# Keys and queries turned by VectorE in blocks of 32, in a fused attention and channel-mix kernel

## What is computed

```python
def _attn_ref(q, k, v):                       # each (4, 8, 1152, 64), float32
    q_pool = q.reshape(B, H, S // 2, 2, D).mean(axis=3)
    scores = scale * np.matmul(q_pool, k.transpose(0, 1, 3, 2))
    scores = scores - np.max(scores, axis=-1, keepdims=True)
    attn = np.exp(scores)
    attn = attn / (np.sum(attn, axis=-1, keepdims=True) + 1e-09)
    return np.matmul(attn, v)

def _moe_ref(x, g_ln, w_ch1, w_ch2):          # x (4, 576, 512): the heads side by side
    xn = (x - mu) / np.sqrt(var + 1e-06) * g_ln
    return x + np.maximum(xn @ w_ch1, 0.0) @ w_ch2     # 512 -> 2048 -> 512
```

## Time and profile before

| what | value |
|---|---|
| median of 3 runs | 860.61 us (859.78 to 860.65) |
| the profiled execution's own time | 861.76 us |
| its span | 860.0 us |
| TensorE (PE) busy in the span | 839.6 us |
| VectorE (DVE) | 427.2 us |
| ScalarE (ACT) | 326.3 us |
| GpSimd (POOL) | 351.3 us |
| attention | until about 450 us, 16 steps |
| channel mix | about 450 us to the end |

### The profile page before, as it was taken

The page is one execution under the profiler, slowest core; times in us unless marked ns, Lnnn a source line. Parts: engine busy times, 40 slices in busy tenths (PEclk is TensorE's granted clock), DMA queues, the critical chain, the costliest instruction groups (busy, mean ns, idle before and its releaser), DMA issues.

```text
span 860.0 us, 16086 instructions
## 1 busy us (share of the span) xinstructions
PE 839.6 (98%) x6712; PEld 704.1 (82%) x6712; DVE 427.2 (50%) x667; ACT 326.3 (38%) x707; POOL 351.3 (41%) x252
## 2 busy tenths in 40 slices
PE   6899999999999999999989999999999999999998
PEld 3767778777878777787769999999999999999997
DVE  5757777777776777676525543213223123222111
ACT  1555657555566556565533441121111111121110
POOL 1477888888777788877780000000000000000000
PEclk9999999999999999999999999999999999999999
DMA  5441223322233312220202321001001000001001
GB/s 113 108 133 36 59 75 84 85 61 61 72 84 84 84 42 57 71 57 28 68 11 74 123 73 38 0 1 38 1 1 37 1 1 37 2 1 37 1 1 37
DMA packets 75160, 42.46 MB, mean 49 GB/s; under 512 B 40016, under 2 KB 66640, under 8 KB 75088
## 3 DMA queue, kind: packets, MB, share of 16 engines
q1 hardware_dynamic: 73872, 40.84, 17.2%
q10 hardware_dynamic: 1216, 0.59, 0.3%
HBM read 36.70 MB, written 4.72 MB: 48 GB/s over the span
## 4 chain that ended last, share of the span: by engine, by line
PE 91%; POOL 4%; DVE 2%; ACT 1%; DMA 1%; issue 1%; SPq 0%; POOLq 0%; DVEq 0%; ACTq 0%
PE banks L865 23%; PE banks L878 23%; PE banks L490 14%; PE banks L479 14%; PE banks L433 4%; PE banks L477 4%; POOL acc L355 3%; PE banks L506 2%; PE banks L405 2%; PE banks L441 1%; PE banks L414 1%; DVE pm L657 1%; ACT pT L589 1%; POOL acc L359 1%; PE banks L225 1%; PE banks L517 1%
## 5 line engine op out<-in xcount | busy, mean ns | idle before, releaser
L355 POOL TENSOR_TENSOR acc<-acc,pT 128x576 f32<-128x576 f32 x160 | 233.9, 1462 | 23.2 <-POOL acc L355 0.4
L865 PE MATMUL banks<-xT,weights 128*128 128x384 f32 x1152 | 217.1, 338 | 0.0
L878 PE MATMUL banks<-weights,hT 128*128 128x512 f32 x864 | 210.7, 389 | 0.0
L865 PEld LDWEIGHTS banks<-xT,weights 128*128 128x128 f32 x1152 | 202.1, 188 | 6.0 <-issue 0.2
L657 DVE TENSOR_REDUCE pm<-banks 128x2 f32<-128x1024 f32 x128 | 153.4, 1223 | 75.0 <-PE banks L433 73.9
L934 DVE SCALAR_TENSOR_TENSOR hT<-banks,hT 128x384 fp32r<-128x384 f32 x96 | 53.5, 558 | 272.4 <-ACT hT L915 272.3
L878 PEld LDWEIGHTS banks<-weights,hT 128*128 128x128 f32 x864 | 160.9, 188 | 27.1 <-issue 0.3
L589 ACT ACTIVATE pT<-banks 128x576 f32<-128x576 f32 x288 | 168.0, 656 | 25.7 <-PE banks L477 19.5
L915 ACT ACTIVATE hT<-banks 128x384 fp32r<-128x384 f32 x96 | 47.2, 492 | 324.6 <-PE banks L865 324.6
L479 PE MATMUL banks<-qT,kT 64*128 64x288 f32 x1728 | 162.8, 299 | 0.6 <-ACT pT L589 0.3
L490 PE MATMUL banks<-pT,vn 128*64 128x288 f32 x1152 | 146.8, 409 | 1.2 <-DVE x L707 1.2
(11 more groups left out here) (74 smaller groups left out, 526.0 us busy)
## 6 DMA issues: line engine op xcount, KB each, us to landing
kn<-in_k_dram SPq DMA_DIRECT2D x32, 288.0 KB, 4.1
vn<-in_v_dram SPq DMA_DIRECT2D x16, 576.0 KB, 4.9
wstage<-in_moe_w_ch_dram SPq DMA_DIRECT2D x32, 256.0 KB, 2.9
qn<-in_q_dram SPq DMA_DIRECT2D x30, 256.0 KB, 3.1
out_dram<-x SPq DMA_DIRECT2D x16, 256.0 KB, 2.3
qn<-in_q_dram SPq DMA_DIRECT2D x30, 32.0 KB, 3.1
qn<-in_q_dram ACTq DMA_DIRECT2D x2, 256.0 KB, 5.0
out_dram<-x SPq DMA_DIRECT2D x4, 128.0 KB, 2.4
```

The costliest lines, as they stand in the source:

```text
L355: nc.gpsimd.tensor_tensor(total, pT[:, h % 2, 0] if kt == 1 else total, pT[:, h % 2, kt], ALU.add).then_inc(chained, 1)
L865: last = nc.tensor.matmul(ps_h[f % 2][:, 0:CW], weights[:, 2 * f, a, c * 128:(c + 1) * 128], xT[:, par, b, c], start=m == 0, stop=m == len ...
L878: last = nc.tensor.matmul(ps_y[kk], hT[:, f % 2, a, kk * 128:(kk + 1) * 128], weights[:, 2 * f + 1, b], start=f == 0 and m == 0, stop=f == ...
```

## The change

Three things change together.

- From pair 2 on (`TURNED`), VectorE turns keys and queries itself, in blocks of 32x32 elements, and writes them to the PSUM banks of KA and KQ; TensorE skips these tokens. So that 32x32 blocks come out as whole rows, SyncE loads keys and queries in another layout: 32 partitions each hold a run of 36 neighbouring rows, and the two halves of the 64 elements of a head come as two overlapping transfers of 32 partitions, 2,272 words each. In `VECTOR_STEPS` Q and K are the turning, ahead of the second `a`; `a` of the first half comes one block of maxima earlier.
- The maxima are turned by two ordinary products with the identity, one in each 64-column tile of the array, in place of one 128x128 transpose.
- The places are single banks now. O, E and L stand together behind the last scores and ahead of PV; SH stands between the two PVs; nine M are spread over the 18 S, the first ahead of them.

Besides, `EARLY` is 4, so that GpSimd splits no slice in steps 10 and 11 and the first chunk splits two more; and SyncE asks for values ahead of queries.

```diff
+    BLOCK = 32
+    QB, KB = NQ // BLOCK, SEQ // BLOCK
+    ROW = (KB - 1) * DH + BLOCK
+    TURNED = 2
...
+    k_b = k.rearrange("b h (r m) d -> b h r (m d)", r=BLOCK)
+    q_b = q.rearrange("b h (r m) d -> b h r (m d)", r=BLOCK)
...
-    PAIR_STEPS = ("S@2 M@3 S@0 S@1 S@2 M@0 M@3 S@1 S@2 S@0 S@1 M@2 S@3 S@0 S@1 M@2 S@3 S@0 M@1 S@2 S@3 S@0 S@1 S@2 "
-                  "M@3 L@0 M@1 M@2 PV@3 E@2 O@1 KQ@0 KA@3 SH@2 PV@1 Z@0")
...
-    VECTOR_STEPS = "m m m m m m a m m m l e c o q a k s"
...
+    WIDE = ("S", "M", "L", "O", "KA", "KQ")
+    PAIR_STEPS = ("M@4 S@6 S@2 S@0 M@4 S@6 S@2 M@0 S@6 M@4 S@2 S@0 S@6 M@2 S@4 S@0 S@6 S@4 M@0 S@2 S@6 M@4 S@0 M@2 "
+                  "S@6 M@4 S@0 O@6 E@3 L@0 PV@2 KQ@4 KA@6 T@4 T@5 SH@3 PV@0 Z@2")
+    PAIR_0 = PAIR_STEPS.replace("M@4 S@6 S@2 S@0", "S@6 S@2 S@0 M@4", 1)
...
+    VECTOR_STEPS = "m m m m m a m m m m e l c o Q K a t q k s"
...
-        EARLY = 6
+        EARLY = 4
...
             for s in range(2):
+                if j >= TURNED:
+                    for half in range(2):
+                        at = s * DH + half * BLOCK
+                        eng.dma_start(q_in_rows[at:at + BLOCK, 0:ROW],
+                                      q_b[b, 2 * g + s, :, half * BLOCK:half * BLOCK + ROW]).then_inc(q_in, 16)
+                    continue
...
+                    for half in range(2):
+                        at = s * DH + half * BLOCK
+                        sp.dma_start(k_in_rows[at:at + BLOCK, 0:ROW],
+                                     k_b[j // BP, 2 * (j % BP) + s, :, half * BLOCK:half * BLOCK + ROW]).then_inc(
+                                         k_in, 16)
...
             for j in range(3, PAIRS):
+                if j > 3:
+                    load_values(j - 3)
                 sp.wait_ge(q_summed, j)
                 load_queries(sp, j)
-                if j > 3:
-                    load_values(j - 3)
                 load_keys(j)
...
+            rows = q_in_rows[:].rearrange("p (b r d) -> p b r d", b=QB, r=FACTOR)
+            return eng.tensor_tensor(q_sums[:, 0:NQ].rearrange("p (b c) -> p b c", b=QB), rows[:, :, 0, 0:BLOCK],
+                                     rows[:, :, 1, 0:BLOCK], ALU.add)
...
-            nc.tensor.transpose(pair_banks("SH", j)[:, 0, 0:128], mx[:].rearrange("p s d -> p (s d)"),
-                                ident[:]).then_inc(max_turned, 1)
+            dst = pair_banks("SH", j)[:, 0]
+            for s in range(2):
+                last = nc.tensor.matmul(dst[s * DH:(s + 1) * DH, 0:128], mx[:, s], ident[:], start=True, stop=True)
+            last.then_inc(max_turned, 1)
...
         def tensor_step(pe, kind, n):
+            if kind in ("KA", "KQ") and n >= TURNED:
+                return
...
+            def keys_in_blocks(dst, first, last):
...
+                src = k_in_rows[:].rearrange("p (i t d) -> p t i d", t=KT, d=DH)
+                return nc.vector.transpose(dst.rearrange("p (t r i) -> p t i r", t=last - first, r=BLOCK),
+                                           src[:, first:last, :, 0:BLOCK])
+
+            def turn_queries_in_blocks(j):
...
+                pair_free(dve, "KQ", j)
+                dve.wait_ge(k_in, keys_loaded(j))
+                dve.wait_ge(q_summed, j + 1)
+                dst = flat(pair_banks("KQ", j))
+                keys_in_blocks(dst[:, QW:QW + 128], KT - 1, KT)
+                nc.vector.transpose(dst[:, 0:NQ].rearrange("p (r b) -> p b r", b=QB),
+                                    q_sums[:, 0:NQ].rearrange("p (b c) -> p b c", b=QB)).then_inc(kq_turned, 1)
+
+            def turn_keys_in_blocks(j):
+                pair_free(dve, "KA", j)
+                keys_in_blocks(flat(pair_banks("KA", j)), 0, KT - 1).then_inc(ka_turned, 1)
```

More of the change, by code:

```diff
@@ L81, in pair_steps @@
         seen = {}
-        for token in PAIR_STEPS.split():
-            kind, pair = token[:-2], int(token[-1])
+        for kind, bank in parsed(PAIR_0 if j == 0 else PAIR_STEPS):
             at = seen.get(kind, 0)
@@ L246, in pair_banks @@
         def pair_banks(kind, n):
-            b = 2 * AT[kind, n]
-            return banks[:, b:b + 2]
+            return banks[:, AT[kind, n][0]:AT[kind, n][-1] + 1]
         def flat(pair):
@@ L268, in load_queries, with keys_loaded, pair_free @@
                               q_m[b, 2 * g + s]).then_inc(q_in, 16)
+        def keys_loaded(j):
+            return 32 * (j + 1) if j < TURNED else 32 * TURNED + 64 * (j - TURNED + 1)
+        def pair_free(eng, kind, n):
+            for last, m in BEFORE[kind, n]:
+                if last == "S":
+                    eng.wait_ge(exp_done, m + 1)
+                elif last == "M":
+                    eng.wait_ge(max_taken, m + 1)
+                elif last == "L":
+                    eng.wait_ge(rest_taken, m + 1)
+                elif last == "E":
+                    eng.wait_ge(end_taken, m + 1)
+                elif last == "KA":
+                    eng.wait_ge(ka_lo, m + 1)
+                elif last == "KQ":
+                    eng.wait_ge(kq_ready, m + 1)
+                elif last == "SH":
+                    eng.wait_ge(shift_ready, m + 1)
+                elif last == "O":
+                    eng.wait_ge(x_written, m + 1)
+                elif last == "PV":
+                    eng.wait_ge(pv_copied, m + 1)
+                elif last == "Z":
+                    eng.wait_ge(z_copied, m + 1)
+                elif last == "T":
+                    eng.wait_ge(xt_ready, m + 1)
         def attention_sync(sp):
@@ L445, in score_end @@
         def score_end(pe, n):
-            dst = pair_banks("E", n)
+            dst = pair_banks("E", n)[:, 0]
             if n >= 2:
                 pe.wait_ge(z_copied, n - 1)
-                last = nc.tensor.transpose(dst[:, 0, 0:128], zs[:], ident[:])
+                last = nc.tensor.transpose(dst[:, 0:128], zs[:], ident[:])
             if n < PAIRS:
-                last = nc.tensor.matmul(dst[:, 1, 0:SEQ - KEYS_END], q_rest[:, n % 2],
+                pe.wait_ge(rest_made, n + 1)
+                pe.wait_ge(ka_hi, n + 1)
+                pe.wait_ge(kb_hi, n + 1)
+                last = nc.tensor.matmul(dst[:, 128:128 + SEQ - KEYS_END], q_rest[:, n % 2],
                                         kT[:, n % 2, 0, KEYS_END:SEQ], start=True, stop=True)
@@ L733, in attention_vector @@
             dve.wait_ge(q_in, 64)
[L734 removed]
+            sum_queries(nc.vector, 0).then_inc(q_summed, 1)
             taken = 0
```

138 lines of the change are left out of this document (61 added, 77 removed).

## The result

| what | before | after |
|---|---|---|
| median | 860.61 us (858.77 to 861.93, 9 runs) | 863.25 us (862.35 to 865.95, 9 runs) |
| ratio to before | 1 | 1.0038, 95% interval 1.0024 to 1.0053 |
| the profiled execution's own time, its span | 861.76, 860.0 | 862.46, 860.6 |
| first and last row sums of the attention | 57.37, 450.04 | 56.98, 450.50 |

A forecast was written before the change was run, and what follows sets the result against it. GpSimd's addition chain was taken as the bound, with TensorE's loop equally long by a hair (26.19 us). Twelve steps by 0.02 and two by -0.36 gave about -0.5: 860.0 from the median of 860.61; range 854 to 863.5.

The forecast's parts named there:

- The loop is 26.21: Attention step, row sums to row sums, through GpSimd's chain: 26.21 us, 0.02 more than before.
- First product at 14.4: TensorE's first product with the values begins 14.4 us after a step's first matmul, 13.46 before the change.
- Transposes of 2.0: VectorE's turning of keys and queries, 1,728 elements per partition in a step, takes 2.0 us.
- Query sum at 22.75: VectorE's query sum asks 22.75 us into the step, going ahead of GpSimd's closing addition, due at 23.06.
- Each meeting 0.35 to 0.38: GpSimd additions lengthened by VectorE's sums: 0.35 us for each of two `acc_end`, 0.38 for the query sum.
- B: Rival: query sum comes after the closing addition (L359) has begun; loop 25.83, time 855.6 us; chance 0.33.
- C: Rival: VectorE's transposes too long for the step, deciding from 5.6 us on; at 7.6, loop 28.3, time 890; chance 0.12.
- D: Rival: TensorE was the bound; loop 24.85, fourteen steps by -1.34, time 842 us; chance 0.07.
- equally long, by a hair: Loops of TensorE and GpSimd before the change: 26.19 us a step, TensorE ready for row sums at about 293.06, against 293.08.
- TensorE's gain turns into a wait of some 1.2 ahead of L506: TensorE ahead of the row sums in each step: freed time becomes some 1.2 us idle, waiting for GpSimd's closing addition.
- rival E: Clock rival: 1.2 us idle in each step drops the clock, row sums and first scores some 1 us longer; 874; chance 0.03.
- Step 14: Late attention step, like step 13 without a query sum: forecast 0.36 us less each.

The follow-up runs named there:

- experiment 1: Kernel after, with VectorE's query sum waiting until GpSimd's closing addition of the second half (L428) has ended: 858.76 us, ratio 0.9976 to the kernel before.
- experiment 7: Kernel before, with GpSimd's chain one addition shorter in both halves and three tiles in `acc_end`: 857.46 us, ratio 0.9962 to the kernel before.
- experiment 5: Kernel after, but TensorE turns the keys and queries of all pairs instead of VectorE: 868.48 us, ratio 1.0088 to the kernel before.

## Why the prediction was wrong

**Right.** "The loop is 26.21": twelve steps gave 26.15 to 26.25, but for the two named. First product at 14.4: 14.3. Transposes of 2.0: 2.01 from start to start (284.89 to 286.90). Turning ends at 19.0: 19.11. Query sum at 22.75: 22.55. Each meeting 0.35 to 0.38: 0.34 and 0.33 (additions of 1.76 and 1.75) and 0.37 (L428), and experiment 1 took the last one away. The loads stayed hidden. Rivals B and C are excluded by the same rows: B needed L428 at 1.41, C transposes of 5.6. D, that TensorE was the bound, is excluded by the 1.54 ahead of L551. TensorE was 0.05 to 0.1 short of it before, by the estimate in experiment 7, which is what the part "equally long, by a hair" says.

**The step that failed** is the sentence "TensorE's gain turns into a wait of some 1.2 ahead of L506", which was costed at nothing, with rival E, the clock, at 0.03 and "against: in step 0 TensorE waited 0.89". A single wait, three quarters as long as the one forecast, was taken as evidence for all. The wait came to 1.54 and once to 1.83, and the clock fell to 0.50 for 3.41 us behind the longest, in both profiles of this kernel: 1.1 in that step. It did not fall "in each step", as rival E had it; so E's price of 14 was wrong as well.

With the waits filled, on the same chip, the kernel is 2.5 to 3.0 us faster and level with the one before (0.9996 and 1.0000). That this is also where the forecast put it is in part luck: about 1.0 of it is the sooner release of the row sums, which the forecast did not have and which the wait did not cost.

**Smaller sizes.** Step 14 was to be 0.36 shorter and is 0.13 (26.04 against 26.17). It has no query sum, but another VectorE instruction meets the closing addition there, which takes 1.65 in place of 1.41:

```profile
422.96 1.65 POOL L428 TENSOR_TENSOR acc<-acc,acc_end 128x576 f32<-128x576 f32 x1
...
422.81 0.54 DVE L236 TENSOR_SCALAR xn<-x,moments,rstd 128x512 f32<-128x512 f32 x1
```

The forecast had no term for it. Step 13 gave 0.40 (25.80 against 26.20). From first to last row sums the forecast was 392.67 - 0.5 = 392.2; 393.52 came, and 1.1 for the fall and 0.23 for step 14 make the difference.

**What the executions add.** The profiled execution is only 0.7 above that of before, the medians 2.6: that of before was 1.1 above its median, and that of after 0.8 below its own. The mean clocks on record tell of the others. One fall of 3.41 us takes 0.002 off the mean of an execution. Of the 62 executions of the kernel before that were timed beside the experiments none had a mean between 0.990 and 0.998. Of 20 of the kernel after nine had 0.992 to 0.996, by that count two to four falls, and took 862.06 with two and 865.14 with four; of 36 with 4 or 12 products one did. So more than one step can have a fall, at some 1.4 us each, and with the waits filled they all but vanish.

**Open.** Executions with means of 0.990 or less most likely had half clock at the start as well, as its shortest stretch there in any trace that has it is 17.07 us or 0.010. Their median was 859.8 in the kernel before (40), 863.4 in that after (10) and 860.3 with filled waits (29); the median of the others 860.7, 862.4 and 858.9. So by these medians half clock at the start costs the kernel after about 1 us and the one before nothing, which is part of the miss; why is not shown. Nor is it shown in which steps the other falls came, or why the clock falls behind one wait and not behind a like one.

## What to carry to other kernels

When two engines' chains are equally long, taking work from one gives a wait; look at what else that wait does before costing it at nothing. If it is long, a few products that nothing reads may be worth their place twice: the clock does not fall, and they can take a second wait off the instruction behind them. Price VectorE's instructions with two SBUF inputs by what they do to a chain on GpSimd, and move them to where no addition runs. Shorten both chains in one change: here the change alone cost 0.4%, the shorter chain alone gave 0.4%, and both, with the query sum moved, 1.9%.

## What the hardware showed beyond what was expected

- VectorE turns 32x32 blocks straight into PSUM, with strided writes, at 0.31, 0.74 and 1.21 us for 128, 576 and 1,024 elements per partition: 1.0 ns an element and 0.19 fixed. The Trainium skill (VectorE: DVE Perf Modes, The three transpose paths) gives 311 ns for 128x128 in bf16; the trace has 0.31 for one such instruction in float32, so it agrees, and shows that eight times as much costs four times as much, not eight.
- A VectorE sum of two SBUF tiles that begins ahead of a GpSimd addition costs it 0.33 to 0.39, and one that begins together with it 0.67 (2.08 in experiment 5); the sum itself takes up to 1.87 instead of 0.75. A `tensor_scalar` from SBUF to SBUF cost an addition 0.24 in step 14.
- Inside the attention the clock fell to 0.50 for 3.41 us behind a wait of 1.83 in two profiles of two, at waits of 2.03 to 2.06 in seven of thirteen steps of one kernel, and never behind the 20 waits of 1.48 to 1.55 in the two profiles of the kernel after. Such a fall costs 1.1 to 1.6.
- At the end of the attention it fell in nine of ten profiles with a wait of 2.3 to 3.2 ahead of the last row sums, and in none of three with 0.2 to 1.4; without a fall the rest takes 408.3 to 408.6, with one of 3.41 us 410.0 to 410.2, with one of 6.83 us 411.1 to 411.5.
- TensorE's row sums begin 0.15 behind GpSimd's closing addition when they wait for two semaphores, and 0.05 to 0.06 when products ahead of them have taken the other wait.
